# Three buffers instead of two for the weights of a product unit, sums taken a unit earlier, high halves taken at a unit's head

## The reference

```
a   = windowed attention(q, k, v, mem_k, mem_v)        # B=4, H=8, S=768, D=64
x   = a as [3072, 512]
x   = x + gate * relu(x @ w1[e]) @ w2[e]               # a mixture of 8 experts, one per token,
                                                       # only where x @ w_skip > 0
h   = max(max(x @ w1, x @ w2), x @ w3)                 # three 512 x 768 matrices
out = h @ w_out                                        # 768 x 512
```

## Time and profile before

| | |
|---|---|
| median of 3 runs | 755.53 us (752.57 to 757.26) |
| the profiled execution | 757.08 us, span 755.3 us, mean granted TensorE clock 0.975 |
| TensorE matmul | busy 683.5 us, 90% |
| TensorE weight load | busy 559.0 us, 74% |
| VectorE | busy 473.5 us, 63% |
| ScalarE | busy 329.8 us, 44% |
| GpSimd | busy 125.2 us, 17% |
| DMA | 102.57 MB, mean 136 GB/s |

### The profile page before, as it was taken

How to read it: one execution, slowest core, us unless ns; L and a number is a source line. 1 busy time by engine, 2 the same in 40 slices (tenths; PEclk the granted TensorE clock), 3 DMA queues, 4 the chain that set the end, 5 groups by cost and what they waited for, 6 DMA issues and landing times.

```text
span 755.3 us, 13174 instructions
## 1 busy us (share of the span) xinstructions
PE 683.5 (90%) x4903; PEld 559.0 (74%) x4903; DVE 473.5 (63%) x811; ACT 329.8 (44%) x509; POOL 125.2 (17%) x153
## 2 busy tenths in 40 slices
PE   5999957999999999978898999989888999898998
PEld 4677735999999999856676778867666887676786
DVE  5777767666666666568777684266667626667530
ACT  4455423555555555454444353333344523434321
POOL 7311113244454544500000000000000000000000
PEclk9999976999999999999999999989999999999999
DMA  8998925765656655560110114101011110110011
GB/s 308 410 327 290 362 98 194 231 223 201 201 206 221 214 184 199 188 218 33 56 56 28 56 56 165 59 28 56 28 57 33 65 70 28 57 56 28 29 42 71
DMA packets 34548, 102.57 MB, mean 136 GB/s; under 512 B 5644, under 2 KB 5772, under 8 KB 34384
## 3 DMA queue, kind: packets, MB, share of 16 engines
q1 hardware_dynamic: 30640, 96.04, 36.5%
q0 software_dynamic: 3296, 5.00, 1.9%
q10 hardware_dynamic: 576, 1.05, 0.4%
HBM read 89.20 MB, written 16.79 MB: 140 GB/s over the span
## 4 chain that ended last, share of the span: by engine, by line
PE 47%; DMA 4%; issue 4%; ACT 3%; DVE 2%; POOL 0%; SPq 0%; ACTq 0%; DVEq 0%; POOLq 0%
PE ps_c L1332 8%; PE ps_c L1334 7%; PE ps_c L1333 7%; PE ps_b L1332 4%; PE ps_b L1333 4%; PE ps_b L1334 4%; PE ps_f L1332 2%; PE ps_f L1333 2%; PE ps_f L1334 2%; DMA u_f<-wunit 2%; ACT f_u L607 2%; PE ps_a L1333 1%; PE ps_a L1332 1%; PE ps_a L1334 1%; DMA x_in<-x_dram,idx_g 1%
## 5 line engine op out<-in xcount | busy, mean ns | idle before, releaser
L1332 PE MATMUL ps_c<-c_hi,u_lo 128*128 128x512 f32 x216 | 88.5, 410 | 41.2 <-ACT f_u L607 38.8
L987 DVE TENSOR_TENSOR w_lo<-raw,w_hi 128x1024 fp32r<-128x1024 f32 x66 | 82.8, 1264 | 52.8 <-ACT w_hi L646 52.8
L646 ACT ACTIVATE w_hi<-raw 128x1024 fp32r<-128x1024 f32 x67 | 70.9, 1059 | 60.9 <-PE ps_y L1334 50.5
L1334 PE MATMUL ps_c<-c_hi,u_hi 128*128 128x512 f32 x216 | 85.9, 398 | 0.0
L1333 PE MATMUL ps_c<-c_lo,u_hi 128*128 128x512 f32 x216 | 85.7, 397 | 0.0
L1332 PEld LDWEIGHTS ps_c<-c_hi,u_lo 128*128 128x128 f32 x216 | 41.2, 191 | 59.9 <-ACT f_u L607 48.5
L636 ACT ACTIVATE u_hi<-u_f 128x1792 fp32r<-128x1792 f32 x27 | 45.9, 1698 | 65.4 <-DVE u_f L1006 65.4
L1332 PE MATMUL ps_h<-x_hi,w_lo 128*128 128x256 f32 x256 | 72.9, 285 | 0.2 <-DVE w_lo L987 0.2
L1333 PE MATMUL ps_h<-x_lo,w_hi 128*128 128x256 f32 x256 | 72.7, 284 | 0.0
L1334 PE MATMUL ps_h<-x_hi,w_hi 128*128 128x256 f32 x256 | 72.7, 284 | 0.0
L1010 DVE TENSOR_TENSOR u_lo<-u_f,u_hi 128x1792 fp32r<-128x1792 f32 x27 | 54.7, 2025 | 18.6 <-ACT u_hi L636 14.4
(11 more groups left out here) (217 smaller groups left out, 1483.7 us busy)
## 6 DMA issues: line engine op xcount, KB each, us to landing
raw<-wpack SPq DMA_DIRECT2D x67, 512.0 KB, 3.7
u_f<-wunit SPq DMA_DIRECT2D x27, 512.0 KB, 3.3
v_sb<-vW SPq DMA_DIRECT2D x32, 390.0 KB, 5.3
k_sb<-kT SPq DMA_DIRECT2D x32, 250.0 KB, 4.9
q_sb<-qT SPq DMA_DIRECT2D x16, 384.0 KB, 5.7
x_dram<-x_buf SPq DMA_DIRECT2D x4, 1536.0 KB, 10.6
out<-f_out SPq DMA_DIRECT2D x24, 256.0 KB, 2.0
f_in<-x_dram SPq DMA_DIRECT2D x2, 2048.0 KB, 9.2
```

The costliest lines, as they stand in the source:

```text
L646: act.activation(w_hi[c % RING][:, :], raw[:, c % RAW, :], ACT.Copy).then_inc(s_whi, 1)
L987: dve.tensor_tensor(w_lo[c % RING][:, :], raw[:, c % RAW, :], w_hi[c % RING][:, :].bitcast(F32), ALU.subtract).then_inc(s_wlo, 1)
L1332: pe.matmul(out_, a_lo, b_hi, start=first, stop=False, skip_group_check=goes_on)
L1334: return pe.matmul(out_, a_hi, b_hi, start=False, stop=end, skip_group_check=goes_on)
```

## The change

The two buffers `u_f` and `u_lo` become three (UBUF). Each buffer is indexed by n % UBUF; `u_hi` stays at two. The output buffer `f_out` goes from 4 to 2 places. SP loads unit n+3 after unit n, and two units instead of one ahead of `w_out`. On VectorE, `unit_low(n+1)` moves ahead of `quarter_11(n)`, and behind it stand the sums of unit n+2 instead of those of n+1. On ScalarE, `unit_high(n+1)` moves ahead of `copy_p1(n)` and gets a wait of its own for the products of unit n-1.

```diff
-OUTS = 4
+OUTS = 2
+UBUF = 3
...
-            u_f = [sb(f"u_f{i}", [P, 8, KH * P]) for i in range(2)]
+            u_f = [sb(f"u_f{i}", [P, 8, KH * P]) for i in range(UBUF)]
...
-            u_lo = [sb(f"u_lo{i}", [P, 8, KH * P], F32R) for i in range(2)]
+            u_lo = [sb(f"u_lo{i}", [P, 8, KH * P], F32R) for i in range(UBUF)]
...
-            load_unit(1)
+            for n in range(1, UBUF):
+                load_unit(n)
             sp.dma_start(o_f[:, :, :], wout).then_inc(s_oload, 16)
...
-                    if n + 2 < NG * UNITS:
+                    if n + UBUF < NG * UNITS:
                         sp.wait_ge(s_prod, n * 7 + 7)
-                        load_unit(n + 2)
+                        load_unit(n + UBUF)
...
             def unit_high(n):
+                if n >= 2:
+                    act.wait_ge(s_prod, n * 7 - 7)
                 act.wait_ge(s_usum, n * 4 + 4)
...
             def unit(g, u):                               # ScalarE
-                copy_p1(n, s)
                 if n + 1 < NG * UNITS:
                     unit_high(n + 1)
+                copy_p1(n, s)
                 copy_u2(n, s)
...
                 if u >= 1:                                # VectorE, unit(g, u)
                     quarter_21(n - 1)
-                if 0 < n < NG * UNITS - 1:
-                    unit_sums(n + 1)
-                if n > 0:
-                    quarter_11(n)
                 if n + 1 < NG * UNITS:
                     unit_low(n + 1)
-                if n == 0:
-                    quarter_11(n)
+                quarter_11(n)
+                if n + 2 < NG * UNITS:
+                    unit_sums(n + 2)
```

More of the change, by code:

```diff
@@ L327, in build @@
         s_landed = sem("s_landed")
-        s_uload = [sem(f"s_uload{i}") for i in range(2)]
+        s_uload = [sem(f"s_uload{i}") for i in range(UBUF)]
         s_oload = sem("s_oload")
@@ L409, in load_unit @@
             def load_unit(n):
-                sp.dma_start(u_f[n % 2][:, 0:4, :], wunit[n % UNITS].rearrange("p (b c) -> p b c", b=4))\
-                    .then_inc(s_uload[n % 2], 16)
+                sp.dma_start(u_f[n % UBUF][:, 0:4, :], wunit[n % UNITS].rearrange("p (b c) -> p b c", b=4))\
+                    .then_inc(s_uload[n % UBUF], 16)
             sp.dma_start(q_sb[0][:, :], qT[0, 0]).then_inc(s_qk[0], 16)
@@ L634, in unit_high @@
             def unit_high(n):
+                if n >= 2:
+                    act.wait_ge(s_prod, n * 7 - 7)
                 act.wait_ge(s_usum, n * 4 + 4)
-                act.activation(u_hi[n % 2][:, :, :], u_f[n % 2][:, 1:8, :], ACT.Copy).then_inc(s_uhi, 1)
+                act.activation(u_hi[n % 2][:, :, :], u_f[n % UBUF][:, 1:8, :], ACT.Copy).then_inc(s_uhi, 1)
             act.wait_ge(s_table, 1)
@@ L997, in unit_sums @@
             def unit_sums(n):
-                w = u_f[n % 2]
-                dve.wait_ge(s_uload[n % 2], n // 2 * 16 + 16)
+                w = u_f[n % UBUF]
+                dve.wait_ge(s_uload[n % UBUF], n // UBUF * 16 + 16)
                 dve.tensor_tensor(w[:, T1, :], w[:, B12, :], w[:, B11, :], ALU.subtract).then_inc(s_usum, 1)
@@ L1009, in unit_low @@
                 dve.wait_ge(s_uhi, n + 1)
-                dve.tensor_tensor(u_lo[n % 2][:, 1:8, :], u_f[n % 2][:, 1:8, :], u_hi[n % 2][:, :, :].bitcast(F32),
+                dve.tensor_tensor(u_lo[n % UBUF][:, 1:8, :], u_f[n % UBUF][:, 1:8, :], u_hi[n % 2][:, :, :].bitcast(F32),
                                   ALU.subtract).then_inc(s_ulo, 1)
@@ L1375, in product @@
             def product(bank, c, b, n, first):
-                w = n % 2
                 for k in range(KH):
-                    last = three(bank[:, :], u_hi[w][:, b - 1, k * P:(k + 1) * P], u_lo[w][:, b, k * P:(k + 1) * P],
+                    at = slice(k * P, (k + 1) * P)
+                    last = three(bank[:, :], u_hi[n % 2][:, b - 1, at], u_lo[n % UBUF][:, b, at],
                                  c_hi[:, c, k, :], c_lo[:, c, k, :], first and k == 0, k == KH - 1, not first)
```

## The result

The changed kernel takes 709.52 us (median of 4 runs, 708.43 to 712.80) against 755.89 us for the one before (4 runs): a ratio of 0.940, interval 0.9356 to 0.9443. The profiled execution took 709.68 us; the forecast was 711, with a range of 706.4 to 722.

What follows compares the result with a forecast made beforehand. TensorE was held by a ScalarE copy behind high halves, sums and load; 52.3 - 1.6 (unit 1) - 3.5 (ten short waits) - 1.0 (gather) = 46.2 us off 757.08 gave 711 us, range 706.4 to 722.

Steps and rivals of the forecast that it cites:

- What bounded the kernel: Unit stages: TensorE waits for a ScalarE copy behind high halves, sums and load; unit 4 loses 2.02 us.
- a landing of about 8 us: SP's unit loads: each may take about 8 us before TensorE notices; loads landed within 6.4 us.
- The excess of 52.3 us: Unit stages from unit 1: 299.81 us for 26 units against 247.52 without waits.
- the two new terms: Head of units: 1.6 us lost in unit 1, and ten short waits before product 3, 0.35 us each, 3.5 us.
- its four falls: Unit stages: four stretches of lower clock behind waits, some 1.5 us each, expected to go with the waits.
- VectorE's chain: VectorE's work per unit closes within the unit: 8.6 us of 9.52, costing nothing.
- The gather: Last expert block: 512 KB more loaded ahead of `w_out` delays the gather by 1.0 us, bounds 0 and 2.1.
- The stores: Two output places: each copy waits for the store two back, cover 8.2 us against 2 us landing; no cost.

Runs made afterwards that it cites:

- E7: The changed kernel with each unit load held back by 3 more products inside a group; 709.54 us, ratio 0.942.
- E8: The changed kernel with each unit load held back by 5 more products inside a group; 760.29 us in one run.
- E4: The changed kernel with ScalarE's first copy back ahead of the high halves, sums still a unit early; 706.51 us, ratio 0.9345.
- E6: The changed kernel with ScalarE's first copy first, `quarter_11` ahead of the low halves, unit 2's load behind the first rows' loads; 705.85 us, ratio 0.9361.
- E1: The changed kernel with both old orders, on ScalarE and VectorE, keeping three weight places and two output places; 708.57 us, ratio 0.9392.
- E5: The changed kernel run again unchanged, in the second series; 710.77 us, ratio 0.9427.
- E3: The kernel before with 2 output places instead of 4 and nothing else; 753.53 us, ratio 0.9986.
- E2: The kernel before, two weight places, with only ScalarE's high halves moved ahead of the first copy and their own wait added; 873.67 us in one run.

## Why the prediction was right

**What bounded the kernel** was read rightly: TensorE behind a copy, the copy behind the high halves, these behind the sums, the sums behind the load. E7 and E8 show the last link: delaying the load by three products costs nothing, by five everything. I had put the limit at a landing of about 8 us into the unit. E7's loads mostly land 7.5 to 8.2 us into it. E8's land at 10.7 in units 10 and 19, which are hardly late themselves, and mostly at 12.1 to 12.4 in the late units, whose fifth product is late as well.

**The excess of 52.3 us and its sign.** It shrank to 5.0: 1.6 in unit 1 (11.15 - 9.52, forecast 1.56) and ten times 0.34 (forecast 0.35). These are the two new terms, at the places named. 52.3 - 5.0 = 47.3, measured 47.2 between the marks. E4 and E6 confirm the 52.3: without any wait there the same stretch takes 310.37 us in both, 52.3 less than the 362.62 before.

**Luck** lies in the part ahead of these marks. Unit 1's mark came at 348.6 us before and at 348.5 in the changed kernel's profile, but between 345.7 (E7) and 352.9 (E8) in the others. Two single executions could have differed by several us more or less than the 47.4 that they did; that the forecast came within 1.5 us of the measured time is partly this.

**The clock.** I counted its four falls, some 6 us, as a part of the gain. The steps between matmuls are 0.43 us instead of 0.23 in a fall, and the four cost 1.6 to 1.7 us each, 6.5 us. In the stages of the units there is none in the profiles of the changed kernel, E1, E4, E5, E6 and E7, whose waits from unit 2 on are short. It comes back with the waits: 3 falls among E8's 21 waits of 1.7 us, 3 in E3's 23, 4 in the 23 before, and one at each of the 23 waits of 4.5 us in E2. That the falls go with the waits is shown; why only some waits of 2 us bring one is open.

**VectorE's chain** closes as worked out. Its timeline in unit 5, whose first matmul starts at 387.14: low halves, `quarter_11`, sums, `quarter_22`:

```profile
389.18 2.02 DVE L1014 TENSOR_TENSOR u_lo<-u_f,u_hi 128x1792 fp32r<-128x1792 f32 x1
391.12 0.68 DVE L1068 TENSOR_TENSOR f_p<-ps_a,f_p 128x512 f32<-128x512 f32 x1
...
392.44 0.41 DVE L1004 TENSOR_TENSOR u_f<-u_f 128x256 f32<-128x256 f32 x1
...
394.84 0.69 DVE L1068 TENSOR_TENSOR f_p<-f_u,f_p 128x512 f32<-128x512 f32 x1 [0.85 <-ACT f_u L609]
```

They start 2.0, 4.0, 5.3 and 7.7 us into the unit, the forecast's numbers. E7 shows that the cover is larger than its sum suggests: sums that start 2.0 to 3.6 us later change nothing.

**The gather** is the term that was mis-sized. I took 1.0 us, between 0 and 2.1, because the gather and `w_out` ended together. With the load ahead of `w_out` TensorE's wait was 0.81 to 1.18 us in five profiles of six, against 0 to 1.17 in the four without it; the medians of E5 and E6 leave nothing for it either. In the changed kernel's profile `w_out` landed at 316.92, and TensorE had gone on with the gathered rows at 313.89: they no longer ended together, so the common end had said nothing about cause. The rule of the Trainium skill that I set against the row ("DMA: Bandwidth & Descriptors", "Queues, rings and completion order", turns between queues by packet) spoke for 0, and these profiles fit it, but for the 2.00 us of E8. With 0 the forecast would have been 710.

**The stores** cost nothing, as E3 shows. The cover was a little smaller than I worked out, though: a store is issued 0.6 us after its copy starts, so 7.5 of the 8.2 us are left. In E4's profile a store behind the 2 MB row load took 8.0 us to land and held a copy until 459.42. TensorE didn't wait for it.

**What the prediction didn't ask** is which part earns the gain. E1 answers: the third place alone, with the loads it lets start sooner. The new orders together add nothing on top (0.9392 against 0.940), since with the load landed in time VectorE made the sums almost in time anyway. Taken singly they cancel. Between the marks of units 1 and 26 E1 takes 313.54 us, E4 310.37 and the changed kernel 315.37: the new order on VectorE gains 3.2 us, nearly all in the first group, and the new place of the high halves costs 5.0, the ten short waits and unit 1. The medians of E1 and E4, 708.57 and 706.51, point the same way, but their intervals overlap. The parts aren't independent, though: ScalarE's order without the third place costs 119 us (E2), and early sums with the old order on ScalarE give the best version.

What differs most between profiles now is the part up to unit 1. From unit 0's mark to unit 1's it takes 14.9 to 15.1 us when the clock stays full (E1, E7), 16.5 when it falls for about 3.4 us (the changed kernel, E5, E6) and 17.7 in E4's profile, where it falls for 6.8. E4's profile had already reached unit 0's mark 2.6 us later than E1's. So the profile of E4 (708.04) is slower than that of E1 (706.13), though its unit stages are the shorter ones. Medians have to be compared, not profiles.

## What to carry to other kernels

Follow a chain of waits to its last link before reordering anything: here three engines waited in a row, and only the start of a transfer mattered. A buffer that lets it start a unit sooner did nearly all of the work; a reorder on an in-order engine then only moved the wait, and had to be paid for where one more instruction stood ahead of a copy that TensorE needs.

Sum the loss from start times of equal units, not from the wait rows: the rows said 38.8 us, the start times 52.3, since restarts and the slower clock behind a wait aren't in the rows, and the rows of the matmuls hid ten of the eleven new waits.

## What the runs showed of the hardware that I had not expected

- The clock's price grows faster than the wait. Waits of about 1.7 us brought a fall in 3 or 4 of 21 to 23 cases, 1.6 to 1.7 us each. Waits of 4.5 us brought one in all 23, mostly 2.6 us each, so E2's mean granted clock was 0.904 against 0.975.
- A matmul that restarts behind a short wait costs 0.11 us beyond the wait: the second step is 0.34 us instead of 0.23, whether the wait was 0.2 us (changed kernel, unit 4) or 1.9 us. Where the clock is already down at the restart, as in most units of E2, it is 0.59.
